# Attention and two expert layers on one core: when the fifth and sixth weight slices are split, the SBUF order behind it, the first loads and the warm-up count

## The chip, the core and the metric

The kernel runs on one core of a Trainium2 chip. TensorE (PE) does the matmuls and writes PSUM; VectorE (DVE), ScalarE (ACT) and GpSimd (POOL) do the elementwise work; SyncE (SP) issues nearly all of the DMAs. Each engine runs its own instruction stream in order, and they wait for each other by semaphores. The metric is the time of the device for one execution, in microseconds (us); lower is better.

## What is computed

Attention over 2 batches, 8 heads, 768 positions and 64 dimensions, in which a query sees only the keys that fall in the same bucket (6 sign bits of a projection), and then two dense blocks (each in, activation, out) on the 1536 x 512 result. All is float32; w_in is 512 x 2048 and w_out 2048 x 512.

```python
def _attn_ref(q, k, v, proj) -> np.ndarray:
    ...
    mask = q_bucket[:, :, :, None] == k_bucket[:, :, None, :]
    scores = scale * np.matmul(q, k.transpose(0, 1, 3, 2))
    scores = np.where(mask, scores, -1000000000.0)
    ...
    attn = attn / (np.sum(attn, axis=-1, keepdims=True) + 1e-09)
    return np.matmul(attn, v).astype(np.float32)

def _moe_ref(x, w_in, w_out) -> np.ndarray:
    h = x @ w_in
    alpha = 1.0
    g = np.where(h > 0.0, h, alpha * (np.exp(np.minimum(h, 0.0)) - 1.0))
    return (g @ w_out).astype(np.float32)
...
def _moe2_ref(x, w_in, w_out, s, b) -> np.ndarray:
    h = x @ w_in
    r = np.maximum(h, 0.0)
    g = s * (r * r) + b
    return (g @ w_out).astype(np.float32)
```

## The kernel before

Precision is kept by splitting every float32 operand into a rounded high part and a low remainder (`_hi`, `_lo`) and running three matmuls in place of one.

**Attention** goes over 8 pairs of heads (`PAIRS`), each pair over 12 units of 128 queries (`UNITS`). A unit is: scores on PE (L623, L624), scaling on DVE (L893), exp on ACT (L787), transposes on PE (L637), the high part by ACT (L781) and the low part by DVE (L900); every third unit goes through `pt_raw` and is split on POOL (`split_third`, L454 and L456). The product with the values (`times_v`, L652 and L653) runs in four groups of a pair (`GROUPS`). Its result takes a way of its own: DVE copies it out of PSUM (`keep_x`, L921; for groups 2 and 3 into `x_second`), SP moves it across partitions by DMA (`move_first` L339, `move_second` L346), POOL adds the two parts (`sum_x`, L463), scales them by the inverse row sums and splits them into `xt_hi` and `xt_lo` (`split_x`, L473, L476, L478). That is done for each of the two halves n of a pair, and POOL does half 1 of a pair during the next pair.

**Dense layers** go over 3 chunks of 512 tokens (`CHUNKS`), each over 16 slices f of the hidden dimension (`FT`). `hidden(layer, c, f)` is 12 matmuls of 512 columns (L672), `output(layer, c, f)` 12 more (L690); ACT and DVE make the activation in between. In the very first chunk `chunk(0, 0, 2, 3)` runs `output` three slices behind `hidden`, and slices 0 and 1 have had their `hidden` inside the attention's last pair. PE waits in `hidden` for `w_split >= f + 1`.

**Weights.** Slice f arrives by two DMAs of 256 KB (`load_w`, L317 and L318) in one of two buffers `w_raw`, and POOL splits it (`split_w`, L496 and L498; called by `weights(f)`). A load of slice f waits until slice f - 2 is split. Slices 0 to 3 (`EARLY = 4`) go to tiles of their own, `wa_hi` and `wa_lo`. Slices 4 and up go to `wb_hi` and `wb_lo`, which lie over memory of the attention: tiles are laid out in the order in which the program names them, `att.close()` gives the attention's region back, and `wb_*` are named after it. From L122 on that region holds, in KB per partition, `raw` 0 to 6, `qqk` to 33, `pt_hi` to 51, `pt_lo` to 69, then the row sums, `kt1`, `probs` and the rest. `wb_hi` begins at 24 and `wb_lo` at 72, 4 KB a slice. So slice 4 lies over `qqk` and `kt1`, operands of the scores, and POOL waits for the last scores (`scores_done`, L526) before it writes there.

What sets the order around this is nothing but the order in which the streams of POOL and SP are written. At the end of the last pair (i = 7) POOL does slice 4 before `split_x(6, 1)`, and slice 5 between the two halves of pair 7. SP issues the load of slice 4 ahead of `move_first(7, 1)`, and that of slice 5 ahead of the two `move_second` of pair 7.

**Start.** SP loads the table of planes (26 KB) and then the first half of head 0's rows, ACT the second half. PE runs `keep_warm(WARM)`, seven matmuls on zeros, then `first_signs` (L593: one float32 matmul of 44 x 384 outputs for each half of the rows, recorded as four instructions; it waits for `planes_built` and `rows0_in`), eight more warm-up matmuls, and the first scores. Between `first_signs` and the scores DVE turns the signs into bits (`to_bits`, L881).

Of the kernel before, what the change touches and what calls it, by code (L numbers as in the profile page):

```python
# [7 lines left out]
F32 = mybir.dt.float32  # L8
F32R = mybir.dt.float32r
# [3 lines left out]
P = 128  # L13
BATCH, HEADS, SEQ, DH = 2, 8, 768, 64
BITS = 6
BIT_ROWS = 32
TILES = SEQ // P
HALF = SEQ // 2
# [12 lines left out]
W = 2 * DM  # L31
WARM = 7

# [62 lines left out]
def build(nc, qk, v, planes_in, ident_in_d, w1_in, w1_out, w2_in, w2_out, s2, b2, out, inv_d):  # L96
    ctx = ExitStack()
    with ctx:
# [3 lines left out]
        def sb(name, shape, dt, where=ctx):  # L102
            return where.enter_context(nc.sbuf_tensor(name, shape, dt))
# [21 lines left out]
        qt1, qt2, kt2 = [[t[:, m, :] for t in qqk] for m in range(3)]  # L125

        pt_hi = [sb(f"pt_hi{n}", [P, TILES, HALF], F32R, att) for n in range(2)]
        pt_lo = [sb(f"pt_lo{n}", [P, TILES, HALF], F32R, att) for n in range(2)]

        row_sum = sb("row_sum", [P, UNITS, 2], F32, att)  # L130
        row_min = sb("row_min", [P, UNITS], F32, att)
        row_inv = sb("row_inv", [P, UNITS], F32, att)
        kt1 = [sb(f"kt1_{n}", [P, SEQ], F32R, att) for n in range(SETS)]

        probs = [sb(f"probs{n}", [P, SEQ], F32, att) for n in range(SRING)]
        raw_v = [sb(f"raw_v{n}", [P, TILES, DH], F32, att) for n in range(2)]
        pt_raw = sb("pt_raw", [P, SEQ], F32, att)
        bits = sb("bits", [SIGN_ROWS, HALF], F32R, att)
# [5 lines left out]
        ones = sb("ones", [P, HT], F32, att)  # L144
        v_nat = [sb(f"v_nat{n}", [P, TILES, 2 * DH], F32R, att) for n in range(2)]

# [117 lines left out]
        def _(sp):  # L264
# [49 lines left out]
            def load_w(layer, f, buf, splits):  # L314

                wait(sp, w_split, splits)
                sp.dma_start(w_raw[buf][:, 0:DM].rearrange("p (c n) -> p c n", n=P), row(win_d[layer], f)).then_inc(w_landed[buf], 16)  # L317
                sp.dma_start(w_raw[buf][:, DM:W], row(wout_d[layer], f)).then_inc(w_landed[buf], 16)  # L318
# [29 lines left out]
            def pair(i):  # L348
# [41 lines left out]
                get_inv(i, 0)  # L390
                if not nxt:
                    load_w(0, EARLY, 0, EARLY - 1)
                move_first(i, 1)
                put_inv(i, 3)

            sp.dma_start(planes_in_sb[:], planes_in).then_inc(planes_landed, 16)
            sp.dma_start(raw[0][:, halves[0]], qk[0, :, halves[0]]).then_inc(rows0_in[0], 16)
# [7 lines left out]
            for i in range(PAIRS):  # L405
                pair(i)
                if i == 1:
                    sp.dma_start(sb_scale[:, 0:1], s2.rearrange("(a n) -> a n", a=1).to_broadcast([P, 1])).then_inc(scale_in, 16)
                    sp.dma_start(sb_scale[:, 1:2], b2.rearrange("(a n) -> a n", a=1).to_broadcast([P, 1])).then_inc(scale_in, 16)
            load_w(0, EARLY + 1, 1, EARLY)  # L410
            move_second(PAIRS - 1, 0)
            move_second(PAIRS - 1, 1)
            get_inv(PAIRS - 1, 1)


            with sp.Fori(EARLY // 2 + 1, FT // 2) as j:
                for n in range(2):
                    load_w(0, 2 * j + n, n, 2 * j + n - 1)
# [21 lines left out]
        def _(pool):  # L440
# [62 lines left out]
            def pair(i, place, prev=True, nxt=True):  # L503
# [19 lines left out]
                split_third(i, 3)  # L523
                if not nxt:

                    pool.wait_ge(scores_done, UNITS * PAIRS)  # L526
                    pool.nop(nofuse=True)
                    weights(EARLY)
                if prev:
# [36 lines left out]
            split_x(PAIRS - 1, 0)  # L566
            weights(EARLY + 1)
            sum_x(PAIRS - 1, 1)
            split_x(PAIRS - 1, 1)

            with pool.Fori(1, (FT - EARLY) // 2) as j:
# [207 lines left out]
        def _(act):  # L779
# [29 lines left out]
            def unit(i, k, place, more=True):  # L809
# [12 lines left out]
                if first and k == 1:  # L822
                    round_qk(2, 0, 2, 1)

            act.dma_start(raw[0][:, halves[1]], qk[0, :, halves[1]]).then_inc(rows0_in[1], 16)
            act.wait_ge(ones_ready, 1)
# [214 lines left out]
```

## Time and profile before

| | us |
|---|---|
| median of 3 runs | 756.19 (755.26 to 756.28) |
| time of the profiled execution | 756.28 |
| its span, first to last instruction | 754.5 |

The span is 1.8 us short of the execution's time. Attention takes the first 232 us or so, the two dense layers the rest. In the page's list of chains, PE holds 94% of the chain that ended last; the rest lies mostly on POOL and on weight loads by DMA. In the timelines "idle before" is how long the engine stood still just before that instruction, and "<-" names what ended it.

### The profile page before, as it was taken

How to read it: one execution, taken by the hardware profiler on the slowest of the kernel's cores; microseconds unless marked ns; L12 is line 12 of the kernel's file. 1: busy time of each engine (PE TensorE's matmuls, PEld its weight loads, DVE VectorE, ACT ScalarE, POOL GpSimd, SP SyncE). 2: the span in 40 equal slices, each digit the busy share in tenths (PEclk: the TensorE clock that was granted, in tenths of full speed). 3: DMA queues.
4: the chain of work that ended last, by engine and by line, in shares of the span. 5: the costliest groups of instructions: out<-in, count | busy, mean ns of one | idle time of the engine just before them, and what ended most of it. 6: DMA issues, size and time to landing. Idle time of an engine off the chain costs nothing.

```text
span 754.5 us, 11772 instructions
## 1 busy us (share of the span) xinstructions
PE 746.6 (99%) x3757; PEld 641.6 (85%) x3757; DVE 392.8 (52%) x756; ACT 315.5 (42%) x614; POOL 312.7 (41%) x251
## 2 busy tenths in 40 slices
PE   8999999999999999999999999999999999999997
PEld 6999999999998788888888888888888888888886
DVE  6888888888877564343334232443234323343233
ACT  7888888888873122222123212232222212121211
POOL 6799989988999992000000666620000000000000
PEclk9999999999999999999999999999999999999999
DMA  5765575465533341000000232300001000010001
GB/s 158 186 170 133 129 176 147 115 151 139 128 91 94 111 139 58 0 1 1 0 1 0 84 107 87 100 12 1 0 1 56 0 0 0 0 56 0 0 0 56
DMA packets 44466, 50.67 MB, mean 67 GB/s; under 512 B 8260, under 2 KB 33172, under 8 KB 44436
## 3 DMA queue, kind: packets, MB, share of 16 engines
q1 hardware_dynamic: 44148, 50.02, 24.4%
q8 instruction: 17, 0.28, 0.2%
q10 hardware_dynamic: 288, 0.26, 0.1%
q14 instruction: 13, 0.11, 0.1%
HBM read 29.45 MB, written 3.19 MB: 43 GB/s over the span
## 4 chain that ended last, share of the span: by engine, by line
PE 94%; POOL 3%; DMA 1%; DVE 1%; issue 0%; ACT 0%; SPq 0%; DVEq 0%; POOLq 0%
PE acc L690 34%; PE h_ps L672 32%; PE pt_ps L637 8%; PE s_ps L624 4%; PE s_ps L623 4%; PE pv_ps L652 4%; PE pv_ps L653 4%; POOL wb_lo L498 1%; DMA w_raw<-w_out_dram 1%; PE prep_ps L605 1%; PE prep_ps L604 1%; PE prep_ps L606 1%; PE pv_ps L611 1%; POOL x_sum L473 1%; POOL wb_hi L496 0%
## 5 line engine op out<-in xcount | busy, mean ns | idle before, releaser
L859 ACT ACTIVATE r_sb<-h_ps 128x512 f32<-128x512 f32 x96 | 57.4, 598 | 362.3 <-PE h_ps L672 362.3
L672 PE MATMUL h_ps<-xt_hi,wb_hi 128*128 (+1 forms) x288 | 112.1, 389 | 0.6 <-POOL wb_lo L498 0.6
L672 PE MATMUL h_ps<-xt_hi,wb_lo 128*128 (+1 forms) x288 | 112.0, 389 | 0.0
L672 PE MATMUL h_ps<-xt_lo,wb_hi 128*128 (+1 forms) x288 | 112.0, 389 | 0.0
L992 DVE TENSOR_SCALAR g_sb<-e_sb,sb_scale 128x512 f32<-128x512 f32 x48 | 27.8, 579 | 158.2 <-ACT e_sb L862 158.2
L893 DVE TENSOR_SCALAR_CACHE_REDUCE probs<-s_ps 128x768 f32<-128x768 f32 x96 | 91.8, 957 | 9.6 <-PE s_ps L624 7.1
L990 DVE SCALAR_TENSOR_TENSOR g_sb<-e_sb,h_ps 128x512 f32<-128x512 f32 x48 | 33.0, 687 | 121.8 <-ACT e_sb L862 121.3
L787 ACT ACTIVATE probs<-probs,row_min 128x768 f32<-128x768 f32 x96 | 90.0, 938 | 2.8 <-DVE probs L893 1.9
L637 PE MATMUL pt_ps<-ident_sb,probs 128*128 128x128 f32 x576 | 80.2, 274 | 1.3 <-DVE pt_lo L900 1.0
L998 DVE TENSOR_TENSOR g_lo<-g_sb,g_hi 128x512 fp32r<-128x512 f32 x96 | 74.0, 771 | 3.3
L637 PEld LDWEIGHTS pt_ps<-ident_sb,probs 128*128 128x128 f32 x576 | 68.1, 141 | 7.8 <-issue 2.3
L652 PE MATMUL pv_ps<-pt_hi,v_nat 128*128 128x384 f32 x192 | 72.2, 376 | 0.0
L900 DVE TENSOR_TENSOR pt_lo<-pt_ps,pt_hi 128x384 fp32r<-128x384 f32 x128 | 65.1, 550 | 3.6 <-ACT pt_hi L781 3.4
L623 PE MATMUL s_ps<-kt,qqk 128*128 128x384 f32 x192 | 65.4, 341 | 0.7 <-DVE probs L893 0.5
L624 PE MATMUL s_ps<-qqk 76*128 76x384 f32 x192 | 65.3, 340 | 0.0
L862 ACT ACTIVATE e_sb<-r_sb 128x512 f32<-128x512 f32 x96 | 60.7, 632 | 11.0 <-ACT r_sb L859 0.8
L653 PE MATMUL pv_ps<-pt_lo,v_nat 128*128 128x384 f32 x192 | 64.8, 337 | 0.0
L672 PEld LDWEIGHTS h_ps<-xt_hi,wb_hi 128*128 128x128 f32 x288 | 54.0, 188 | 12.1 <-issue 1.0
L672 PEld LDWEIGHTS h_ps<-xt_lo,wb_hi 128*128 128x128 f32 x288 | 54.1, 188 | 11.2
L672 PEld LDWEIGHTS h_ps<-xt_hi,wb_lo 128*128 128x128 f32 x288 | 54.1, 188 | 11.2
L496 POOL CAST wa_hi<-w_raw 128x1024 fp32r<-128x1024 f32 (+1 forms) x8 | 8.9, 1114 | 131.1 <-PE acc L690 131.1
L781 ACT ACTIVATE pt_hi<-pt_ps 128x384 fp32r<-128x384 f32 x128 | 55.9, 489 | 17.4 <-PE pt_ps L637 17.4
(92 smaller groups left out, 1527.1 us busy)
## 6 DMA issues: line engine op xcount, KB each, us to landing
w_raw<-w_in_dram SPq DMA_DIRECT2D x32, 256.0 KB, 2.8
w_raw<-w_out_dram SPq DMA_DIRECT2D x32, 256.0 KB, 2.9
raw<-qk_dram SPq DMA_DIRECT2D x15, 384.0 KB, 5.7
qqk<-kt SPq DMA_DIRECT2D x15, 384.0 KB, 3.8
raw_v<-v_dram SPq DMA_DIRECT2D x16, 192.0 KB, 4.2
all_inv<-inv_dram SPq DMA_DIRECT2D x16, 192.0 KB
x_parts<-x_second SPq DMA_DIRECT2D x16, 192.0 KB, 5.7
qqk<-qqk SPq DMA_DIRECT2D x15, 192.0 KB, 3.7
```

What stands on the lines that cost most here:

```text
L623: mm(s_ps[buf][:, n, 0:HALF], q1, kt1[ops][:, cols], start=True, stop=False)
L624: last = mm(s_ps[buf][:, n, 0:HALF], q2, kt2[ops][score_rows, cols], start=False, stop=True)
L637: last = nc.tensor.transpose(pt_ps[n][:, r * P:(r + 1) * P], probs[k % SRING][:, (n * HT + r) * P:(n * HT + r + 1) * P], ident_sb[:])
L652: mm(pv_ps[:, 0:HALF], v_nat[par][:, kt, :], pt_hi[buf][:, kt, :], start=kt == 0, stop=False)
L653: last = mm(pv_ps[:, 0:HALF], v_nat[par][:, kt, :], pt_lo[buf][:, kt, :], start=False, stop=kt == TILES - 1)
L672: last = mm(bank[:], w[a][:, kt * P:(kt + 1) * P], x[b], start=n == 0, stop=n == 3 * KT - 1)
L690: last = mm(acc[n][:], lhs, rhs, start=f == 0 and j == 0, stop=f == FT - 1 and j == 2)
L787: nc.scalar.activation(scores[:], scores[:], ACT.Exp, bias=row_min[:, k:k + 1], scale=-1.0, accum_out=row_sum[:, k, 0:1]).then_inc(exp_don ...
L862: nc.scalar.activation(e[:], r[:], ACT.Square if layer else ACT.Exp, scale=1.0 if layer else -1.0).then_inc(e_done, 1)
L893: ts(probs[k % SRING][:].rearrange("p (n c) -> p n c", n=2), s_ps[k % 2][:, :, 0:HALF], -SCALE, CEILING, ALU.mult, ALU.min, accum_out=row_ ...
L900: tt(pt_lo[(k // HT) % 2][where], pt_ps[n][:, 0:HALF].rearrange("p (t c) -> p t c", t=HT), pt_hi[(k // HT) % 2][where].bitcast(F32), ALU.s ...
L998: tt(lo[:], g[:], hi[:].bitcast(F32), ALU.subtract).then_inc(g_ready, 1)
```

## The change

- POOL: `weights(4)` leaves the end of the last pair and comes after `split_x(7, 0)`, and it waits for `pv_done`, the last product with the values, in place of `scores_done`. `weights(5)` comes after `split_x(7, 1)`.
- SP: the load of slice 4 comes after `move_second(7, 0)`, that of slice 5 after `get_inv(7, 1)`.
- SBUF: the order of the attention's tiles is another. `kt1`, `raw_v`, `v_nat`, `bits` and the planes come behind `qqk`, and `probs`, `pt_raw`, `pt_hi` and `pt_lo` behind those. Slice 4 in `wb_lo` (72 to 76 KB) then lies over `pt_hi`, an operand of `times_v`. No size changes.
- The load of the planes is issued by ACT, ahead of its half of the rows, and no longer by SP ahead of the other half.
- `WARM` is 10, from 7.

```diff
@@ -29,7 +29,7 @@
 END = 384
 CHUNKS = TOKENS // CHUNK
 W = 2 * DM
-WARM = 7
+WARM = 10
 
 EARLY = 4
 HBANKS, GRING, SRING = 4, 3, 3
@@ -123,18 +123,9 @@
 
         qqk = [sb(f"qqk{n}", [P, 3, SEQ], F32R, att) for n in range(SETS)]
         qt1, qt2, kt2 = [[t[:, m, :] for t in qqk] for m in range(3)]
-
-        pt_hi = [sb(f"pt_hi{n}", [P, TILES, HALF], F32R, att) for n in range(2)]
-        pt_lo = [sb(f"pt_lo{n}", [P, TILES, HALF], F32R, att) for n in range(2)]
-
-        row_sum = sb("row_sum", [P, UNITS, 2], F32, att)
-        row_min = sb("row_min", [P, UNITS], F32, att)
-        row_inv = sb("row_inv", [P, UNITS], F32, att)
         kt1 = [sb(f"kt1_{n}", [P, SEQ], F32R, att) for n in range(SETS)]
-
-        probs = [sb(f"probs{n}", [P, SEQ], F32, att) for n in range(SRING)]
         raw_v = [sb(f"raw_v{n}", [P, TILES, DH], F32, att) for n in range(2)]
-        pt_raw = sb("pt_raw", [P, SEQ], F32, att)
+        v_nat = [sb(f"v_nat{n}", [P, TILES, 2 * DH], F32R, att) for n in range(2)]
         bits = sb("bits", [SIGN_ROWS, HALF], F32R, att)
         planes_in_sb = sb("planes_in_sb", [P, C_END], F32, att)
         planes0 = sb("planes0", [P, 2, BIT_ROWS], F32, att)
@@ -142,7 +133,15 @@
         planes_hi = sb("planes_hi", [P, 2 * SIGN_ROWS], F32R, att)
         planes_lo = sb("planes_lo", [P, 2 * SIGN_ROWS], F32R, att)
         ones = sb("ones", [P, HT], F32, att)
-        v_nat = [sb(f"v_nat{n}", [P, TILES, 2 * DH], F32R, att) for n in range(2)]
+
+        probs = [sb(f"probs{n}", [P, SEQ], F32, att) for n in range(SRING)]
+        pt_raw = sb("pt_raw", [P, SEQ], F32, att)
+        pt_hi = [sb(f"pt_hi{n}", [P, TILES, HALF], F32R, att) for n in range(2)]
+        pt_lo = [sb(f"pt_lo{n}", [P, TILES, HALF], F32R, att) for n in range(2)]
+
+        row_sum = sb("row_sum", [P, UNITS, 2], F32, att)
+        row_min = sb("row_min", [P, UNITS], F32, att)
+        row_inv = sb("row_inv", [P, UNITS], F32, att)
 
         all_inv = [sb(f"all_inv{n}", [P, HALF], F32, att) for n in range(2)]
 
@@ -388,12 +387,9 @@
                 if nxt:
                     copy_q_lo(2 * i + 3)
                 get_inv(i, 0)
-                if not nxt:
-                    load_w(0, EARLY, 0, EARLY - 1)
                 move_first(i, 1)
                 put_inv(i, 3)
 
-            sp.dma_start(planes_in_sb[:], planes_in).then_inc(planes_landed, 16)
             sp.dma_start(raw[0][:, halves[0]], qk[0, :, halves[0]]).then_inc(rows0_in[0], 16)
             sp.wait_ge(rows0_in[0], 16)
             load_qk(1)
@@ -407,12 +403,13 @@
                 if i == 1:
                     sp.dma_start(sb_scale[:, 0:1], s2.rearrange("(a n) -> a n", a=1).to_broadcast([P, 1])).then_inc(scale_in, 16)
                     sp.dma_start(sb_scale[:, 1:2], b2.rearrange("(a n) -> a n", a=1).to_broadcast([P, 1])).then_inc(scale_in, 16)
-            load_w(0, EARLY + 1, 1, EARLY)
             move_second(PAIRS - 1, 0)
+            load_w(0, EARLY, 0, EARLY - 1)
             move_second(PAIRS - 1, 1)
             get_inv(PAIRS - 1, 1)
 
 
+            load_w(0, EARLY + 1, 1, EARLY)
             with sp.Fori(EARLY // 2 + 1, FT // 2) as j:
                 for n in range(2):
                     load_w(0, 2 * j + n, n, 2 * j + n - 1)
@@ -521,11 +518,6 @@
                 if not prev:
                     weights(0)
                 split_third(i, 3)
-                if not nxt:
-
-                    pool.wait_ge(scores_done, UNITS * PAIRS)
-                    pool.nop(nofuse=True)
-                    weights(EARLY)
                 if prev:
                     split_x(i - 1, 1)
                 else:
@@ -564,9 +556,13 @@
             pair(PAIRS - 1, PAIRS - 1, nxt=False)
             sum_x(PAIRS - 1, 0)
             split_x(PAIRS - 1, 0)
-            weights(EARLY + 1)
+
+            pool.wait_ge(pv_done, GROUPS * PAIRS)
+            pool.nop(nofuse=True)
+            weights(EARLY)
             sum_x(PAIRS - 1, 1)
             split_x(PAIRS - 1, 1)
+            weights(EARLY + 1)
 
             with pool.Fori(1, (FT - EARLY) // 2) as j:
                 for n in range(2):
@@ -822,6 +818,7 @@
                 if first and k == 1:
                     round_qk(2, 0, 2, 1)
 
+            act.dma_start(planes_in_sb[:], planes_in).then_inc(planes_landed, 16)
             act.dma_start(raw[0][:, halves[1]], qk[0, :, halves[1]]).then_inc(rows0_in[1], 16)
             act.wait_ge(ones_ready, 1)
             nc.scalar.activation(row_sum[:, 0, 0:1], ones[:, 0:1], ACT.Exp)
```

The places in the streams, from before and from the change. POOL at the end of the last pair, before (the number after a tile's name is its buffer: `x_sum1` is half 1, `w_raw0` holds slice 4, `w_raw1` slice 5):

```order
L496 CAST wb_hi<-w_raw0 128x1024 [waits scores_done,w_landed0]
L498 TENSOR_TENSOR wb_lo<-w_raw0,wb_hi 128x1024 [waits w_hi]
L473 TENSOR_TENSOR x_sum1<-x_sum1,all_inv1 128x384 [waits x_summed,inv_in1]
L476 CAST xt_hi<-x_sum1 128x384 [waits x_scaled]
L478 TENSOR_TENSOR xt_lo<-x_sum1,xt_hi 128x384 [waits xt_hi_done]
L463 TENSOR_TENSOR x_sum0<-x_parts0 128x384 [waits second_moved0]
L473 TENSOR_TENSOR x_sum0<-x_sum0,all_inv0 128x384 [waits x_summed,inv_in0]
L476 CAST xt_hi<-x_sum0 128x384 [waits x_scaled]
L478 TENSOR_TENSOR xt_lo<-x_sum0,xt_hi 128x384 [waits xt_hi_done]
L496 CAST wb_hi<-w_raw1 128x1024 [waits w_landed1]
L498 TENSOR_TENSOR wb_lo<-w_raw1,wb_hi 128x1024 [waits w_hi]
L463 TENSOR_TENSOR x_sum1<-x_parts1 128x384 [waits second_moved1]
```

And in the change:

```order
L470 TENSOR_TENSOR x_sum1<-x_sum1,all_inv1 128x384 [waits x_summed,inv_in1]
L473 CAST xt_hi<-x_sum1 128x384 [waits x_scaled]
L475 TENSOR_TENSOR xt_lo<-x_sum1,xt_hi 128x384 [waits xt_hi_done]
L460 TENSOR_TENSOR x_sum0<-x_parts0 128x384 [waits second_moved0]
L470 TENSOR_TENSOR x_sum0<-x_sum0,all_inv0 128x384 [waits x_summed,inv_in0]
L473 CAST xt_hi<-x_sum0 128x384 [waits x_scaled]
L475 TENSOR_TENSOR xt_lo<-x_sum0,xt_hi 128x384 [waits xt_hi_done]
L493 CAST wb_hi<-w_raw0 128x1024 [waits pv_done,w_landed0]
L495 TENSOR_TENSOR wb_lo<-w_raw0,wb_hi 128x1024 [waits w_hi]
L460 TENSOR_TENSOR x_sum1<-x_parts1 128x384 [waits second_moved1]
L470 TENSOR_TENSOR x_sum1<-x_sum1,all_inv1 128x384 [waits x_summed,inv_in1]
L473 CAST xt_hi<-x_sum1 128x384 [waits x_scaled]
```

The two rows of slice 4 have moved behind both `split_x(6, 1)` and the whole of half 0 of pair 7, and those of slice 5 (no longer in the piece) behind half 1.

SP at the same place, before, from the last `get_inv(7, 0)` on:

```order
L333 DMA all_inv0<-inv_dram 128x1x384 [waits x_scaled,inv_out0]
L317 DMA w_raw0<-w1_in_dram 128x4x128 [waits w_split]
L318 DMA w_raw0<-w1_out_dram 128x512
L339 DMA x_parts1<-x_parts1 64x384 [waits x_done,x_summed]
L326 DMA inv_dram<-row_inv 128x3 [waits inv_done,inv_in1]
L317 DMA w_raw1<-w1_in_dram 128x4x128 [waits w_split]
L318 DMA w_raw1<-w1_out_dram 128x512
L346 DMA x_parts0<-x_second0 64x2x384 [waits x_done,first_moved0]
L346 DMA x_parts1<-x_second1 64x2x384 [waits x_done,first_moved1]
L333 DMA all_inv1<-inv_dram 128x1x384 [waits x_scaled,inv_out1]
```

And in the change:

```order
L332 DMA all_inv0<-inv_dram 128x1x384 [waits x_scaled,inv_out0]
L338 DMA x_parts1<-x_parts1 64x384 [waits x_done,x_summed]
L325 DMA inv_dram<-row_inv 128x3 [waits inv_done,inv_in1]
L345 DMA x_parts0<-x_second0 64x2x384 [waits x_done,first_moved0]
L316 DMA w_raw0<-w1_in_dram 128x4x128 [waits w_split]
L317 DMA w_raw0<-w1_out_dram 128x512
L345 DMA x_parts1<-x_second1 64x2x384 [waits x_done,first_moved1]
L332 DMA all_inv1<-inv_dram 128x1x384 [waits x_scaled,inv_out1]
L316 DMA w_raw1<-w1_in_dram 128x4x128 [waits w_split]
L317 DMA w_raw1<-w1_out_dram 128x512
```

Two pairs of weight DMAs have changed places with the moves of `x_parts`: slice 4 now stands behind the first `x_second` row, slice 5 behind the last `all_inv` row.

## Rows read from the trace of the kernel before

**Rows 1.** The page: busy time by engine, and the granted clock in 40 slices.

```profile
PE 746.6 (99%) x3757; PEld 641.6 (85%) x3757; DVE 392.8 (52%) x756; ACT 315.5 (42%) x614; POOL 312.7 (41%) x251
...
PEclk9999999999999999999999999999999999999999
```

**Rows 2.** Timeline of the start: start us, us, engine, line, op, tiles, [idle before].

```profile
0.75 0.42 ACTq L825 DMA_DIRECT2D raw<-qk_dram  x1
...
1.21 0.42 SPq L397 DMA_DIRECT2D raw<-qk_dram  x1
...
1.33 2.61 PE L611 MATMUL pv_ps<-pt_hi 128*128 128x384 f32 x7 [1.33 <-DVE pt_hi L945]
...
3.80 0.52 ACT L781 ACTIVATE kt<-raw 64x384 fp32r<-64x384 f32 x1 [1.11 <-DMA raw<-qk_dram]
...
3.91 2.76 PE L593 MATMUL s_ps<-raw,planes 128*44 128x384 f32 x4
...
6.71 2.36 DVE L881 TENSOR_SCALAR qqk<-s_ps,planes_in_sb 12x768 fp32r<-12x768 f32 x3 [1.80 <-PE s_ps L593]
...
8.72 0.41 PE L623 MATMUL s_ps<-kt,qqk 128*128 128x384 f32 x1
```

**Rows 3.** Weight loads of the warm-up matmuls: two of the first seven, the second eight.

```profile
1.82 0.33 PEld L611 LDWEIGHTS pv_ps<-pt_hi 128*128 128x128 f32 x1
...
3.10 0.33 PEld L611 LDWEIGHTS pv_ps<-pt_hi 128*128 128x128 f32 x1
...
L611 PEld LDWEIGHTS pv_ps<-pt_hi x8: 187/188/333, 6.6 to 8.1; 128*128 128x128 f32 x8
```

**Rows 4.** Timeline of POOL (GpSimd) from 212 to 249 us.

```profile
212.57 1.02 POOL L463 TENSOR_TENSOR x_sum<-x_parts 128x384 f32<-128x384 f32 x1
...
216.51 0.53 POOL L488 CAST v_nat<-raw_v 128x384 fp32r<-128x384 f32 x1
...
226.12 1.85 POOL L456 TENSOR_TENSOR pt_lo<-pt_raw,pt_hi 128x768 fp32r<-128x768 f32 x1
...
228.64 1.04 POOL L496 CAST wb_hi<-w_raw 128x1024 fp32r<-128x1024 f32 x1 [0.67 <-DMA w_raw<-w_out_dram]
...
232.12 1.13 POOL L473 TENSOR_TENSOR x_sum<-x_sum,all_inv 128x384 f32<-128x384 f32 x1
...
234.93 1.20 POOL L463 TENSOR_TENSOR x_sum<-x_parts 128x384 f32<-128x384 f32 x1
...
239.69 1.23 POOL L496 CAST wb_hi<-w_raw 128x1024 fp32r<-128x1024 f32 x1
...
243.69 1.19 POOL L463 TENSOR_TENSOR x_sum<-x_parts 128x384 f32<-128x384 f32 x1
...
248.68 1.04 POOL L496 CAST wb_hi<-w_raw 128x1024 f32 x1
```

**Rows 5.** Timeline of SP's DMA issues near the seam.

```profile
228.59 5.40 SPq L346 DMA_DIRECT2D x_parts<-x_second  x2
...
235.60 0.35 SPq L318 DMA_DIRECT2D w_raw<-w_out_dram  x1
```

**Rows 6.** Landing of L346's first of these; of L318's four (220 to 245 us).

```profile
DMA to landing us min/median/max: 3.3/3.3/3.3
...
DMA to landing us min/median/max: 4.5/5.9/6.9
```

**Rows 7.** Timeline of PE: first matmul of hidden steps 4, 5 and 6.

```profile
240.80 0.39 PE L672 MATMUL h_ps<-xt_hi,wb_hi 128*128 128x512 f32 x1
...
246.24 0.39 PE L672 MATMUL h_ps<-xt_hi,wb_hi 128*128 128x512 f32 x1
...
252.43 0.47 PE L672 MATMUL h_ps<-xt_hi,wb_hi 128*128 128x512 f32 x1 [0.59 <-POOL wb_lo L498]
```

**Rows 8.** Busy time of DVE in three stretches: stretch, its length, busy (count), clock, DMA.

```profile
212.50:216.50 4.00, 3.32 (x8) 1.00 0.05 12
...
228.60:232.10 3.50, 0.00 (x0) 1.00 0.48 152
...
240.00:246.00 6.00, 5.90 (x6) 1.00 0.18 54
```

## The prediction

> **What bounds the kernel now.** I read the page first, then the timelines of two short stretches. PE is busy for 746.6 of 754.5 us, and the granted clock stands at full speed in all 40 slices [rows 1]. So a change that adds no matmul in the dense layers can only move the few microseconds in which PE stands still or runs at the slow pace. There are two such places, and the change touches both.
>
> The first is the start. The warm-up matmuls follow each other at the pace of their weight loads, four steps in 1.28 us (1.82 to 3.10), or 0.32 us a matmul of 384 columns [rows 3]. That is 1200 columns per us, the lower of the two levels (1.2 GHz), though the page's row of the clock shows full speed there; the pace decides. The second group begins with a 333 ns load and has a median of 188 [rows 3], so the rise to 2.4 GHz falls into it, some 6 us after the first matmul. `first_signs` lies before it: four instructions in 2.76 us, 3.91 to 6.67 [rows 2]. DVE has been idle for 1.80 us when it takes the signs at 6.71, and the first scores follow at 8.72 [rows 2]. This is a chain without slack from PE's first matmul on.
>
> The second is the seam. Hidden step 5 starts 5.44 us after step 4 (240.80, 246.24), which is one `hidden` and one `output` back to back; step 6 would be due at 251.68 and starts at 252.43 after an idle time of 0.59 that POOL's split of slice 6 ends [rows 7]. So POOL is already 0.75 us late there once, and from 226 us on its rows follow each other almost without a gap [rows 4]. Whatever makes POOL stand still, or puts a weight slice behind other work, shows on PE at this place.
>
> **The seam, step by step.** No POOL instruction is added or removed; the order changes. I price POOL's blocks from the start of one to the start of the next [rows 4]:
> - a weight slice: 3.48 us (228.64 to 232.12) or 4.00 (239.69 to 243.69);
> - `sum_x` and `split_x` of one half: 3.94 (212.57 to 216.51), 4.76 (234.93 to 239.69) or 4.99 (243.69 to 248.68);
> - `split_x` alone: 2.81 (232.12 to 234.93).
>
> The short values fall where DVE is idle (228.60 to 232.10) or busy for 3.32 of 4.00 us with the attention's work; the long ones where it is busy for 5.90 of 6.00 us with the activations of the dense layer [rows 8]. From 233 us on I take the long ones.
>
> Now the new order. POOL ends `split_third` at 226.12 + 1.85 = 227.97 and does `split_x(6, 1)` at once: 230.8. Then it needs `second_moved` of half 0. SP issues that move at 228.59 [rows 5] and it lands 3.3 us later [rows 6], at 231.9. POOL stands still for 1.1 us, where before it had slice 4 to do. Half 0 of pair 7 then takes 4.76: 232.0 to 236.7. The wait for `pv_done` costs nothing: the last product is over before hidden step 2, and PE does `hidden` 2, `hidden` 3 and `output` 0 (2.72 us each, half of 5.44) before 240.80, so by 232.6. The load of slice 4 is now issued behind the first `move_second`, at about 229.2 and 229.8; the slowest landing of its kind, 6.9 [rows 6], gives 236.7, just in time. Slice 4: 236.7 + 4.0 = 240.7, and step 4 is due at 240.80. So that one is met, with 0.1 to spare.
>
> Half 1: its move is issued at 233.4 as before (the second in the row of 228.59, which ends at 233.99) and has landed by 236.8. 240.7 + 4.99 = 245.7. Slice 5 is loaded from where slice 6 was loaded before (235.60 [rows 5]), and lands by 242.5 at the slowest [rows 6]: no wait. DVE runs out of work near 248, since PE gives it none, so I price slice 5 by the distance from the split of slice 6 to the matmul that waited for it, 248.68 to 252.43 [rows 4, 7]: 3.75 with the hand-over. Step 5 starts at 249.45, not 246.24: PE stands still for 3.2 us. What was late before, slice 6, no longer is: POOL ends it near 253.1, and step 6 is due at 249.45 + 5.44 = 254.9. Its load is issued when slice 4 is split (240.7) and has at least 8 us. Slice 7 is loaded from 249.3 on, lands by 256.7 at the slowest, is ready by 260.7 and due at 260.4; by the median landing of 5.9 it is on time. After that POOL needs 4 us a slice against PE's 5.44. The net is 3.2 - 0.75 = **+2.5 us**. Bounds: all blocks short gives 0.1 (below); all long, with slice 7 late as well, 3.2.
>
> **The start.** Three more warm-up matmuls at 0.32 us. The tenth load starts at 3.10 + 3 x 0.32 = 4.06, its matmul one step later, and the array is free for `first_signs` at 4.70, against a start at 3.91 before [rows 2, 3]: **+0.8 us**. The data would be there earlier. The first half of the rows was issued at 1.21 behind the planes and used at 3.80, 2.6 us later; issued at 0.75 it is there at 3.35 [rows 2]. But 3.35 is before 4.70, so this gain of 0.45 us is worth nothing while PE is still warming up. The second half moves back on ACT's queue by 0.45, to 1.2, and lands near 3.8, also before 4.70. ACT's and POOL's own parts of head 0 start 0.45 earlier, and nobody on the chain waits for them. `first_signs` took 2.7 us (3.91 to 6.6, where the second warm-up group starts [rows 3]); from 4.70 on it ends at 7.4, about when the clock rises. Bounds: at most 3 x 0.32 = 0.96; at least -0.5, if the clock rose before `first_signs`.
>
> On that: the trace shows the low pace for some 6 us of nearly unbroken work, through seven warm-up matmuls and all of `first_signs` [rows 2, 3]. The Trainium skill says, in TensorE: Matmul & The Clock Gate, What's actually happening, that the array is throttled by default and sustained activity releases it, and that where the rise falls varies from run to run because the monitor does not start with the kernel. By that page an earlier rise is possible here and would turn +0.8 into -0.5; by the row it is not to be expected, since three more matmuls do not begin earlier, they only push `first_signs` back.
>
> **The SBUF order.** No row prices an address. All tiles keep their size and their 128 partitions, and DVE (52%), ACT (42%) and POOL (41%) have room [rows 1]. I take nothing, within 0.3 us either way. The layout's real price is the wait for `pv_done`, counted above.
>
> **The sum.** 756.28 (the profiled execution: a span of 754.5 and 1.8 around it) + 2.5 + 0.8 = 759.6. The median of the runs is 0.1 lower, so 759.5.
>
> **The rivals.**
> - *The clock rises before `first_signs`.* `first_signs` then takes half of 2.7 us: 4.70 + 1.35 = 6.05, 0.5 ahead of the 6.6 of before. With the seam as forecast: 756.2 + 2.5 - 0.5 = 758.2. For it speaks that PE is busy without a break, against it the 6 us above. Slower still.
> - *Not slower: POOL's blocks at the seam run at their short durations.* Place: POOL from 232.0 to the end of slice 5. 232.0 + 3.94 + 3.48 + 3.94 + 3.48 = 246.84. PE then loses about 0.75 at step 5, which is what it lost at step 6 before. The seam costs 0.1, the whole 0.9: 757.1, within 0.2% of before. It decides at 247.0: each 0.1 us by which slice 5 is ready later costs 0.1. For it: 3.94 was measured while DVE was 83% busy. Against it: both blocks that ran beside the activations took 4.76 and 4.99. The Trainium skill, SBUF — State Buffer, Who interferes with whom, has DVE and GpSimd take turns on a shared pair of ports as an exclusive lock, by which the long blocks return wherever DVE works.
> - *PE's clock falls in the 3.2 us of standing still.* No row shows PE idle for that long inside the kernel. [...] The Trainium skill, TensorE: Matmul & The Clock Gate, What's actually happening, has an idle array put back to the low level.
> - *The change does not reach the path.* If the new order on POOL cost nothing in some way I don't see, only the start would be left: 757.0. It has no mechanism but the second rival's, so no chance of its own.
>
> **How the numbers follow.** Forecast (seam 1.9 to 3.2, start 0.4 to 1.0): 58%, its own range 758.5 to 760.4. Early clock: 12%. Short blocks: 10%. Clock falls: 12%. Something that no row prices (a late load at slice 4, where the margin is 0.1, or addresses): 8%, of which 2 faster, 3 within the band. A measurement of this kernel tells 0.2% (1.5 us) from no change; the band is 754.7 to 757.7. Short blocks and those 3 make 13% for the same, and 2% are left for faster; 85% slower. The range holds the forecast, the early clock, most of the short blocks and most of the clock's fall: 757.2 to 762.2.
>
> **What would show it.** In the profile of the changed kernel: `first_signs` at 4.6 to 4.8 and DVE's L881 (now L877) near 7.5; a wait of about 1 us on POOL before its `sum_x` of pair 7, half 0, ended by the DMA of `x_second`; step 4 on time; an idle time of 2.5 to 3.5 us on PE before hidden step 5, ended by POOL's split into `wb_lo`; none before step 6; and PE's pace after it 0.23 us a matmul, at the high level. Wrong would be: no idle time at step 5 (then the blocks were short), an idle time at step 4 as well (the load of slice 4 landed late), 0.43 us a matmul after the gap (the clock fell), or L881 before 6.7 (the clock rose early).

## The result, and the profile after

| | before | changed |
|---|---|---|
| median, us | 755.93 (755.26 to 756.28, 6 runs) | 760.32 (758.14 to 760.88, 6 runs) |
| profiled execution | 756.28, span 754.5 | 758.45, span 756.7 |
| ratio | | 1.0051, 95% interval 1.0037 to 1.0066 |

The changed kernel is slower by 0.5%, as forecast (759.5, 757.2 to 762.2). But its runs, six timed ones and the profiled one, are not one group. Three (the profiled one among them) took 758.1 to 758.5 us at a mean granted clock of TensorE of 1.000; four took 760.3 to 760.9 at 0.997 or 0.998. The profiled execution belongs to the short group, so its trace can't show what the long ones lost; an experiment below does.

The page of the changed kernel. Busy times are those of [rows 1] within 0.1 us for PE and POOL, DVE has 5 us more in the same 756 instructions, and the granted clock is full in all slices:

```profile
span 756.7 us, 11778 instructions
...
PE 746.7 (99%) x3760; PEld 643.1 (85%) x3760; DVE 397.7 (53%) x756; ACT 315.6 (42%) x614; POOL 312.7 (41%) x251
...
PEclk9999999999999999999999999999999999999999
```

The seam on POOL, which answers to [rows 4] (timeline: start, us, engine, line, op, tiles, idle before; lines are 3 lower than before's):

```profile
226.39 1.84 POOL L453 TENSOR_TENSOR pt_lo<-pt_raw,pt_hi 128x768 fp32r<-128x768 f32 x1
...
228.20 1.14 POOL L470 TENSOR_TENSOR x_sum<-x_sum,all_inv 128x384 f32<-128x384 f32 x1
...
232.29 1.01 POOL L460 TENSOR_TENSOR x_sum<-x_parts 128x384 f32<-128x384 f32 x1 [1.23 <-DMA x_parts<-x_second]
...
236.31 1.50 POOL L493 CAST wb_hi<-w_raw 128x1024 fp32r<-128x1024 f32 x1
...
240.31 1.47 POOL L460 TENSOR_TENSOR x_sum<-x_parts 128x384 f32<-128x384 f32 x1
...
244.99 1.24 POOL L493 CAST wb_hi<-w_raw 128x1024 fp32r<-128x1024 f32 x1
...
248.93 1.23 POOL L493 CAST wb_hi<-w_raw 128x1024 f32 x1
```

POOL ends `split_third` at 228.2, does `split_x(6, 1)`, and then stands still for 1.23 us until the DMA of `x_second` lands. Half 0 takes 4.02 us (232.29 to 236.31), slice 4 takes 4.00, half 1 takes 4.68, slice 5 is done before 248.93.

PE at hidden steps 4, 5 and 6, which answers to [rows 7]:

```profile
241.07 0.39 PE L668 MATMUL h_ps<-xt_hi,wb_hi 128*128 128x512 f32 x1
...
249.12 0.47 PE L668 MATMUL h_ps<-xt_hi,wb_hi 128*128 128x512 f32 x1 [2.45 <-POOL wb_lo L495]
...
254.68 0.39 PE L668 MATMUL h_ps<-xt_hi,wb_hi 128*128 128x512 f32 x1
```

Step 4 is on time. Step 5 was due at 241.07 + 5.44 = 246.51 and starts at 249.12, 2.6 us late, after an idle time of 2.45 that POOL's split ends. Step 6 follows 5.56 later without a wait. It started at 252.43 before: 2.25 us of difference, of which 0.27 were there at step 4 already (241.07 against 240.80). That leaves 2.0 for the seam.

The start, which answers to [rows 2]:

```profile
0.75 0.42 ACTq L821 DMA_DIRECT2D planes_in_sb<-planes_dram  x1
...
1.33 3.57 PE L607 MATMUL pv_ps<-pt_hi 128*128 128x384 f32 x10 [1.33 <-DVE pt_hi L942]
...
3.43 0.52 ACT L777 ACTIVATE kt<-raw 64x384 fp32r<-64x384 f32 x1 [0.25 <-DMA raw<-qk_dram]
...
3.61 0.49 DVE L947 TENSOR_TENSOR planes<-planes_in_sb 128x24 f32<-128x24 f32 x1 [2.31 <-DMA planes_in_sb<-planes_dram]
...
4.83 2.06 PE L589 MATMUL s_ps<-raw,planes 128*44 128x384 f32 x4
...
6.94 2.35 DVE L878 TENSOR_SCALAR qqk<-s_ps,planes_in_sb 12x768 fp32r<-12x768 f32 x3 [1.37 <-PE s_ps L589]
...
8.91 0.43 PE L619 MATMUL s_ps<-kt,qqk 128*128 128x384 f32 x1 [0.40 <-issue]
```

The first half of the rows is there at 3.43, before 3.80. `first_signs` starts 0.92 us later than before (4.83, 3.91), but takes 2.06 us in place of 2.76, and the first scores are only 0.19 late (8.91, 8.72). So this trace has +2.0 at the seam and +0.2 at the start. What makes the long group, and why `first_signs` got shorter, was the question for the experiments.

Every experiment ran beside the kernel before on its chip. On two of the three chips a few runs of most kernels, before's too, took some 4 to 10 us more than the rest (called disturbed below), which widens the intervals there; I give medians, and the undisturbed runs where the number needs them.

### The profile page after: what moved, and what is told of

Its sections match the earlier page's. It is cut to its first block, busy times and chain, and to the rows that moved or that the text cites. A ratio compares the mean times of both kernels' runs of the same rounds, so it can differ in the third digit from the quotient of the medians.

```text
span 756.7 us, 11778 instructions
## 1 busy us (share of the span) xinstructions
PE 746.7 (99%) x3760; PEld 643.1 (85%) x3760; DVE 397.7 (53%) x756; ACT 315.6 (42%) x614; POOL 312.7 (41%) x251
## 4 chain that ended last, share of the span: by engine, by line
PE 96%; POOL 2%; issue 0%; DMA 0%; ACT 0%; DVE 0%; DVEq 0%; POOLq 0%; SPq 0%
PE acc L686 34%; PE h_ps L668 33%; PE pt_ps L633 8%; PE s_ps L619 4%; PE pv_ps L648 4%; PE s_ps L620 4%; PE pv_ps L649 4%; PE prep_ps L602 1%; PE pv_ps L607 1%; PE prep_ps L600 1%; PE prep_ps L601 1%; POOL wb_lo L495 1%; DMA x_parts<-x_second 0%; POOL wb_hi L493 0%; POOL x_sum L460 0%
## 5 line engine op out<-in xcount | busy, mean ns | idle before, releaser
L995 DVE TENSOR_TENSOR g_lo<-g_sb,g_hi 128x512 fp32r<-128x512 f32 x96 | 77.8, 810 | 3.3
```

What stands on the lines that cost most here:

```text
L995: tt(lo[:], g[:], hi[:].bitcast(F32), ALU.subtract).then_inc(g_ready, 1)
```

## Experiments

### The seam's part alone

Planes on SP and 7 warm-up matmuls as before; the streams of POOL and SP, the SBUF order and the wait as in the change.

```diff
-WARM = 10
+WARM = 7
...
-            act.dma_start(planes_in_sb[:], planes_in).then_inc(planes_landed, 16)
...
+            sp.dma_start(planes_in_sb[:], planes_in).then_inc(planes_landed, 16)
```

> The kernel before with the seam's part of the change alone (streams of POOL and SP, SBUF order, wait for the last product); planes on SP and 7 warm-up matmuls as before. Theory (seam +2.3 us by PE's wait at hidden step 5, start +0.2 to +0.8, and a further 2 us in those runs in which PE's clock falls in the wait): 758.0 us in runs at mean clock 1.0 and 760.1 in runs at 0.997. Rival 1 (the second cluster comes from the start, not from the wait): all runs near 758.0 at clock 1.0. Rival 2 (the seam costs nothing, the start everything): 756.0.

Measured: 759.78 us (median of 5) against 756.26, ratio 1.0039 (1.0025 to 1.0053). One run of 757.66 at clock 1.000, three of 759.35 to 759.90 at 0.997, and one of 760.18 at 1.000 that fits neither. The two groups are there without the start's part, so the seam makes them. This time the profiled execution (759.35) is one of the long group. The windows around PE's wait (stretch, its length, PE busy and count, granted clock, DMA share, GB/s):

```profile
240.00:246.00 6.00, 6.00 (x28) 1.00 0.30 98
...
246.00:249.00 3.00, 0.56 (x3) 0.88 0.00 0
...
249.00:252.00 3.00, 3.00 (x8) 0.55 0.53 175
...
252.00:256.00 4.00, 4.00 (x19) 1.00 0.42 130
```

and its step 5:

```profile
248.73 0.77 PE L669 MATMUL h_ps<-xt_hi,wb_hi 128*128 128x512 f32 x1 [2.44 <-POOL wb_lo L496]
...
249.29 0.63 PE L669 MATMUL h_ps<-xt_lo,wb_hi 128*128 128x512 f32 x1
...
250.15 0.63 PE L669 MATMUL h_ps<-xt_hi,wb_hi 128*128 128x512 f32 x1
...
252.25 0.39 PE L669 MATMUL h_ps<-xt_hi,wb_hi 128*128 128x512 f32 x1
...
252.71 0.39 PE L669 MATMUL h_ps<-xt_hi,wb_lo 128*128 128x512 f32 x1
...
255.65 0.39 PE L669 MATMUL h_ps<-xt_hi,wb_hi 128*128 128x512 f32 x1
```

PE is idle for 2.44 us, and in that wait the granted clock falls: 0.88 on average over 246 to 249, 0.55 over 249 to 252, full again from 252. In step 5 the matmuls start 0.43 us apart (249.29 to 250.15 is two of them), which is 512 columns at 1.2 GHz, and 0.23 apart at the end (252.25 to 252.71 is two), the pace of the higher level, 2.4 GHz. From the start of the first to the start of the last, the twelve take 3.98 us, in the trace of the change 2.62. The fall costs 1.4 us here.

### PE's wait filled with work

Ten matmuls of 512 columns, into the bank that step 5 overwrites:

```diff
+FILL = 10
...
+                bank = h_ps[f % HBANKS]
+                if layer == 0 and isinstance(c, int) and f == EARLY + 1:
+                    for _ in range(FILL):
+                        mm(bank[:], wa_hi[:, 0:P], xt_hi[:, 0:CHUNK], start=True, stop=True)
                 pe.wait_ge(w_split, layer * FT + f + 1)
-                bank = h_ps[f % HBANKS]
```

> The change whole, and in PE's wait ahead of hidden step 5 ten matmuls of 512 columns into the bank that step 5 overwrites (10 x 0.227 = 2.3 us of a wait of 2.5 us). Theory (the slow runs of the change are those in which the clock falls because PE stands still there): every run at 758.2 to 758.8 and mean clock 1.0, none at 760.3. Rival (the clock falls for another reason): the same two clusters, 758.4 and 760.4.

Measured: 758.97 us (5 runs) against 756.26. No run below 0.999, where the change had four of seven. But the forecast of the times was too tight: 758.05, 758.56 and 758.97 are within it or near, 759.71 and 760.35 are not, at a clock of 0.999. Something else made those two longer; the runs don't show what.

The same with eleven matmuls, and beside it the change itself once more, on a third chip:

```diff
-FILL = 10
+FILL = 11
```

> The change with eleven matmuls of 512 columns in PE's wait ahead of hidden step 5 (11 x 0.227 = 2.5 us, the whole wait). Theory (the clock falls because PE stands still): no run below mean clock 0.999, the undisturbed runs at 758.2 to 759. Rival (it falls for another reason): about half of the runs at 0.997.

> The change itself once more, beside the next three on the same chip. Theory: two groups of runs 2 us apart, the longer one at mean granted clock 0.997 or 0.998: 758.2 to 758.6 and 760.3 to 760.9, about half of the runs in each. Rival: one group only, if the first split was chance.

Measured: 758.26 us with the wait filled (12 runs, none below 0.999) and 758.67 for the change (11 runs, three of them at 0.997 or 0.998), against 756.63. The six shortest filled runs are 757.66 to 757.85; three more lie at 758.66 to 758.80, and three above, all at 0.999 or 1.000. The granted clock in the trace with the wait filled, for the stretch in which it fell above:

```profile
246.00:249.00 3.00, 3.00 (x14) 1.00 0.00 0
...
249.00:252.00 3.00, 3.00 (x15) 1.00 0.54 175
```

PE is busy throughout, the clock stays. Without the fall the seam still costs its 2 us: step 5 starts 8.03 us after step 4 (240.27, 248.30) with the wait filled, and 8.05 in the change (241.07, 249.12). The matmuls only keep the clock up. In the first set more than half of the change's runs had fallen (4 of 7), here 3 of 11, so the median lies in the other group; that fits its being 1.7 lower.

### PE's wait made longer

Two more casts on POOL ahead of slice 5, into room that is overwritten later:

```diff
             split_x(PAIRS - 1, 1)
+            for n in range(4, 6):
+                nc.gpsimd.tensor_copy(at(wb_hi, n), wa_hi[:, 0:W].bitcast(F32))
             weights(EARLY + 1)
```

> The change with two more casts on POOL ahead of the split of slice 5 (into room that slices 8 and 9 take later; the result is the same), which makes PE's wait 2.2 us longer, 4.7 in place of 2.5. Theory: the clock falls in every run, all at mean clock 0.997 or below, and the time is 2.2 us over the longer group of the change: 762.6. Rival 1 (the fall has nothing to do with the length of the wait): still half and half, 760.6 and 762.6. Rival 2 (POOL's delay is hidden): as the change.

Measured: 762.87 us (762.51 to 763.37, 5 runs), ratio 1.0079 (1.0056 to 1.0101), and every run at a mean clock of 0.997 or 0.995. Step 5, and the clock around it:

```profile
252.20 0.77 PE L670 MATMUL h_ps<-xt_hi,wb_hi 128*128 128x512 f32 x1 [5.05 <-POOL wb_lo L495]
```

```profile
249.00:252.00 3.00, 0.00 (x0) 0.54 0.00 0
...
252.00:256.00 4.00, 3.80 (x9) 0.50 0.41 131
...
256.00:262.00 6.00, 6.00 (x27) 0.99 0.47 139
```

The wait is 5.05 us, and the clock is low for most of it and for eight of the twelve matmuls behind it. Step 6 follows step 5 by 7.35 us (252.20, 259.55), where it is 5.56 in the change, so this fall costs 1.8. About half of the runs fall with a wait of 2.4 or 2.5 us (16 of 35), all with one of 5.

The count over all kernels, by the wait that their trace shows:

| kernel | PE's wait at the seam, us | runs at a mean clock of 0.998 or less |
|---|---|---|
| before | 0.59 | 3 of 85 (all three above 761 us, disturbed otherwise) |
| slice 6 ahead (below) | none | 0 of 23 |
| the start's part, or one of its two edits (below) | 0.7 to 1.2 | 0 of 34 |
| wait filled | 0.2 or none | 0 of 17 |
| wait for the last product at the old place (below) | 1.8 and 2.2 | 4 of 12 |
| the change | 2.5 | 7 of 18 |
| seam or order alone | 2.4 | 9 of 17 |
| longer wait | 5.05 | 5 of 5 |

Three of the runs counted here (one of the change at 769.03, two of the order alone at 762.25 and 764.64) are disturbed as well, so a fall at the seam is not certain for them.

### Order, addresses and the wait for the last product

First the streams of the change with the SBUF order of before and `scores_done` as the wait. The edit of the wait, against the change (the order of the tiles goes back as well and is not printed):

```diff
-            pool.wait_ge(pv_done, GROUPS * PAIRS)
+            pool.wait_ge(scores_done, UNITS * PAIRS)
```

> The streams of POOL and SP as in the change, but the SBUF order of before and the old wait for the scores; planes and warm-up as before. Theory (order alone costs, neither addresses nor the wait for the last product do): the same as the seam's part alone, 757.7 in undisturbed runs at clock 1.0 and 759.4 to 760.2 at 0.997. Rival (addresses or the wait cost something): shorter than that by the amount.

Measured: 759.92 us (12 runs, several disturbed) against 756.76, ratio 1.0035 (1.0004 to 1.0066). The two shortest runs are 757.49 and 757.52 at 1.000, and four are 759.30 to 759.77 at 0.997: the same two groups as the seam's part alone (757.66; 759.35 to 759.90). The two kernels ran on chips whose before differs by 0.5 us, so times alone would leave that much open. The traces leave less: from the first scores to hidden step 4 it is 232.08 us before and 232.10 in this run, both with the old addresses, and 232.16 in the change and 232.20 in the seam's part alone, with the new ones. PE's wait at step 5 is 2.43 us here, 2.44 in the seam's part. So neither the addresses nor the wait for the last product cost more than some 0.1 us in the change; the order does.

Then the other way round, streams of before, with the SBUF order of the change and the wait that it forces, at the old place:

```diff
+        kt1 = [sb(f"kt1_{n}", [P, SEQ], F32R, att) for n in range(SETS)]
...
+        v_nat = [sb(f"v_nat{n}", [P, TILES, 2 * DH], F32R, att) for n in range(2)]
...
         pt_hi = [sb(f"pt_hi{n}", [P, TILES, HALF], F32R, att) for n in range(2)]
...
-                    pool.wait_ge(scores_done, UNITS * PAIRS)
+                    pool.wait_ge(pv_done, GROUPS * PAIRS)
                     pool.nop(nofuse=True)
                     weights(EARLY)
```

> The kernel before with the SBUF order of the change and, forced by it, the wait for the last product (pv_done) at the old place of slice 4, ahead of split_x(6, 1); streams otherwise as before. Theory: addresses cost nothing; POOL now waits from 228 to 232.9 us where it had slice 4 to do, and everything behind it, slice 5 and 6 too, is 4.2 us later: PE waits at hidden step 5 for about 1.8 us and at step 6 for about 2.6 more, +3.5 to +4 us over before (760), and a further 2 us in runs in which the clock falls. Rival (the wait is hidden, as 0.0 was taken for it in its new place): near before.

Measured: 760.48 us (12 runs) against 756.76, ratio 1.0045 (1.0027 to 1.0063). POOL's wait, and PE's two:

```profile
232.49 1.04 POOL L496 CAST wb_hi<-w_raw 128x1024 fp32r<-128x1024 f32 x1 [5.01 <-PE pv_ps L653]
```

```profile
248.11 0.47 PE L672 MATMUL h_ps<-xt_hi,wb_hi 128*128 128x512 f32 x1 [1.79 <-POOL wb_lo L498]
...
256.02 0.47 PE L672 MATMUL h_ps<-xt_hi,wb_hi 128*128 128x512 f32 x1 [2.20 <-POOL wb_lo L498]
```

POOL loses 5.01 us and PE 4.0, in two waits. This profiled run (761.46) is one of the four in which the clock falls, and the fall comes behind the second wait, when PE is busy again:

```profile
257.02 0.39 PE L672 MATMUL h_ps<-xt_lo,wb_hi 128*128 128x512 f32 x1
...
257.60 0.63 PE L672 MATMUL h_ps<-xt_hi,wb_hi 128*128 128x512 f32 x1
...
258.03 0.63 PE L672 MATMUL h_ps<-xt_lo,wb_hi 128*128 128x512 f32 x1
```

The first matmuls behind the wait (from 256.02) start 0.23 us apart; from 257.60 on they start 0.43 apart. Step 7 follows at 263.19, 7.17 us after step 6, where 5.56 is the distance without a fall: 1.6 us lost.

So the SBUF order is not harmless as such. It costs 3.7 us where slice 4 is still split early, and nothing to speak of once slice 4 has moved behind the last product: of the two ways to live with the new SBUF order, the moved streams are the cheaper one, at about 2 us with the clock up.

### The start

Both edits of the start, without the seam's:

```diff
-WARM = 7
+WARM = 10
...
-            sp.dma_start(planes_in_sb[:], planes_in).then_inc(planes_landed, 16)
...
+            act.dma_start(planes_in_sb[:], planes_in).then_inc(planes_landed, 16)
```

> The kernel before with the start's part alone: planes issued by ACT, 10 warm-up matmuls. Theory: +0.2 to +0.8 us over before, the spread by when the clock rises in each run; no run at mean clock 0.997 and none 2 us longer than the others. Rival 1: two clusters 2 us apart, if the start makes them. Rival 2 (the extra warm-up matmuls bring the clock up earlier): 0.5 us shorter than before.

Measured: 756.92 us (11 runs) against 756.26, +0.7, ratio 1.0008 (0.9999 to 1.0017): no group at 0.997 and no gain. The interval, -0.1 to +1.3 us, holds zero and the forecast of 0.8 alike, so the runs don't settle the amount. Then each edit alone, first the count:

```diff
-WARM = 7
+WARM = 10
```

> The kernel before with 10 warm-up matmuls in place of 7, nothing else. By the sum on record +0.8 us (3 x 0.32 less the slack). Theory after the first traces: the clock rises between 6 and 7.3 us in every run seen, whatever the count, so a later first_signs runs partly at the high level; +0.2 to +0.6 us. Rival (more warm-up, earlier clock): shorter than before.

Measured: 757.69 us (12 runs) against 756.76 on a disturbed chip, ratio 1.0012 (0.9985 to 1.0039). It says nothing by itself. The profiled run (762.37) is one of the disturbed ones, and its trace shows where part of that time goes: PE waits four times, 3.7 us in all, for the DMA that brings the bits into `qqk` (`PE s_ps L623 <- DMA qqk<-bits`), a wait that the trace of before doesn't have. The expectation read the rise of the clock at 6 to 7.3 us in every trace; that was too narrow, as the trace of the start's part (below) has it near 5. Then the planes:

```diff
-            sp.dma_start(planes_in_sb[:], planes_in).then_inc(planes_landed, 16)
...
+            act.dma_start(planes_in_sb[:], planes_in).then_inc(planes_landed, 16)
```

> The kernel before with only the load of the planes moved to ACT; 7 warm-up matmuls. The first half of the rows is there 0.4 us sooner, but the warm-up ends at 3.75 and first_signs started at 3.91 before. Theory: 0.1 to 0.2 us shorter than before, at most 0.45. Rival: longer by 0.4, if the planes land later behind the 192 KB that are issued with them (in the trace of the change DVE took them at 3.61, in that of before at 3.09).

Measured: 756.40 us (11 runs) against 756.26, ratio 0.9999 (0.9990 to 1.0008): no gain. Its trace says why:

```profile
3.31 0.34 SPq L281 DMA_DIRECT2D raw<-qk_dram  x1
...
3.49 0.50 DVE L950 TENSOR_TENSOR planes<-planes_in_sb 128x24 f32<-128x24 f32 x1 [2.19 <-DMA planes_in_sb<-planes_dram]
...
3.92 0.28 DVE L952 TENSOR_TENSOR planes<-planes_in_sb 128x24 f32<-128x24 f32 x2
...
4.05 2.68 PE L592 MATMUL s_ps<-raw,planes 128*44 128x384 f32 x4
```

The rows are there at 3.31, but the planes, used at 3.09 before, are used at 3.49, and DVE's first step on them takes 0.50 us in place of 0.18. `first_signs` starts at 4.05. In the five traces with the start of before and 7 warm-up matmuls it is 3.91 to 4.03, so the move makes it no earlier. Of the two loads that `first_signs` needs, the planes now come last.

What `first_signs` takes differs by trace, with the same instructions. Two traces with 10 warm-up matmuls, of the start's part and of the longer wait:

```profile
4.83 1.52 PE L592 MATMUL s_ps<-raw,planes 128*44 128x384 f32 x4
...
6.28 1.68 PE L610 MATMUL pv_ps<-pt_hi 128*128 128x384 f32 x8
...
8.37 0.41 PE L622 MATMUL s_ps<-kt,qqk 128*128 128x384 f32 x1 [0.41 <-POOL qqk L554]
```

```profile
4.83 2.49 PE L591 MATMUL s_ps<-raw,planes 128*44 128x384 f32 x4
...
7.25 1.68 PE L609 MATMUL pv_ps<-pt_hi 128*128 128x384 f32 x8
...
9.34 0.41 PE L621 MATMUL s_ps<-kt,qqk 128*128 128x384 f32 x1 [0.41 <-issue]
```

It starts at 4.83 in both and takes 1.52 or 2.49 us; the second group starts at 6.28 or 7.25. That is when the pace goes from the lower level to the higher: at the lower one throughout it takes about 2.7 us, as before's trace has it. From what each trace saves against that, I estimate the rise near 5.0 and 7.0 us in these two, and near 4.5 in the earliest, the trace with eleven matmuls in the wait (`first_signs` 4.64, first scores 8.15). Over the six traces with 7 warm-up matmuls the first scores start at 7.88 to 8.85, 8.53 on average, over the seven with 10 at 8.15 to 9.34, 8.78 on average. The three matmuls cost about 0.25 us, below a scatter of 1 us between runs.

### Slice 6 ahead of half 1

The kernel before loses 0.75 us at step 6. Its `split_x(7, 1)` is needed for chunk 1 only, so the slices that chunk 0 waits for can go first:

```diff
             split_x(PAIRS - 1, 0)
             weights(EARLY + 1)
+            pool.wait_ge(pv_done, GROUPS * PAIRS)
+            pool.nop(nofuse=True)
+            weights(EARLY + 2)
             sum_x(PAIRS - 1, 1)
             split_x(PAIRS - 1, 1)
+            weights(EARLY + 3)
-            with pool.Fori(1, (FT - EARLY) // 2) as j:
+            with pool.Fori(2, (FT - EARLY) // 2) as j:
```

> The kernel before with slice 6 split ahead of half 1 of pair 7, and slice 7 behind it; planes and warm-up as before. Theory: the one wait at hidden step 6 goes, -0.75 us; with planes and warm-up changed as well it was 1.3 shorter than before (755.4 against 756.76). Rival (that gain came from the start): as before.

Measured: 755.47 us (754.75 to 756.42, 11 runs) against 756.63, ratio 0.9982 (0.9971 to 0.9993). The gain is 1.2 us where 0.75 was forecast, and the interval (0.5 to 2.2) holds both; in the trace, hidden steps 4 to 7 take 0.85 us less than before. PE's steps 5 to 7 follow each other by 5.44 us, with no wait:

```profile
246.25 0.39 PE L676 MATMUL h_ps<-xt_hi,wb_hi 128*128 128x512 f32 x1
...
251.69 0.39 PE L676 MATMUL h_ps<-xt_hi,wb_hi 128*128 128x512 f32 x1
...
257.13 0.43 PE L676 MATMUL h_ps<-xt_hi,wb_hi 128*128 128x512 f32 x1
```

With the planes on ACT and 6 warm-up matmuls as well:

```diff
-WARM = 7
+WARM = 6
...
-            sp.dma_start(planes_in_sb[:], planes_in).then_inc(planes_landed, 16)
...
+            act.dma_start(planes_in_sb[:], planes_in).then_inc(planes_landed, 16)
```

> The kernel before with slice 6 split ahead of half 1 of pair 7 (and slice 7 behind it), the planes on ACT and 6 warm-up matmuls. Theory: the wait at hidden step 6 (0.59 us idle, 0.75 us late) goes, the start gains 0 to 0.3: 0.7 to 1.0 us shorter than before. Rival (half 1 pushed back makes slice 7 late, or the wait moves to another slice): no gain or longer.

Measured: 755.40 us (12 runs) against 756.76 on a disturbed chip, ratio 0.9990 (0.9965 to 1.0014); eight of the runs are 754.9 to 756.0. The start adds nothing that I can see. The version with slice 6 ahead beats both kernels: before by 0.2% (the ratio above), and the change by 0.4% (755.47 against 758.67 on the same chip).

## Why the prediction was right, and where its terms were off

**The seam.** The mechanism was right in each step: POOL's wait for the move of half 0 (1.1 forecast, 1.23 measured), step 4 on time, PE waiting at step 5 for `wb_lo`, none at step 6, the wait for the last product free. Its size was not: 2.0 us in place of 2.5, and PE idle for 2.45 us, just under the 2.5 to 3.5 that I had named. Two blocks were priced too long: half 0 took 4.02, not 4.76, and half 1 took 4.68, not 4.99. Half 0 ran from 232.3 to 236.3, and DVE's work on the dense layer starts in that time only; "from 233 us on the long ones" was too coarse (DVE was busy for 2.66 of these 4.00 us, in slice 4 behind it for 3.93 of 4.00). Slice 5 took 4.13 with the hand-over, not 3.75: the short price rested on DVE running out of work near 248, and DVE was busy for 3.93 of 4.00 us from 245 to 249.

**The start.** The step that failed is the length of `first_signs`. I read 2.76 us from one trace and kept it. It is at the low pace only until the clock rises, and the rise came anywhere between some 4.5 and 7 us. A later start then shortens it. Of +0.8 about +0.2 is left in the change's trace, +0.25 over thirteen traces, which is within their scatter; DVE took the signs at 6.94, not near 7.5. The runs of the start's part alone (+0.7) don't tell 0.2 from 0.8. The Trainium skill, TensorE: Matmul & The Clock Gate, What's actually happening, says that the rise moves from run to run; these traces agree. I quoted that, and then priced from the one trace all the same. The rival that the clock rises before `first_signs` had 12%. In two of the seven traces with 10 warm-up matmuls (the start's part alone and the eleven matmuls in the wait) it all but came true: `first_signs` took 1.52 and 1.49 us, near half of 2.76, and the first scores came at 8.37 and 8.15, ahead of the 8.72 of before. But with 7 warm-up matmuls one trace has 1.81 us and 7.88, so this is the scatter of the rise and no work of the extra matmuls, and the median of the start's part alone was not shorter. That the data would be there at 3.35 was half right: the rows were, the planes were not.

**The clock's fall.** This was a rival with a chance of 12%. It is in fact a part of what the change does, in 7 of 18 runs, four of the seven in the first set among them. It costs 1.4 us in each of the two traces with one wait of 2.4 us and a fall (seam's part, order alone), 1.6 behind a second wait of 2.2 us and 1.8 behind the wait of 5.05. The range's upper end, 762.2, left room for a dearer fall; no run here shows one. The groups lie about 2 us apart. What makes up the other 0.6 is open: no run of the change's long group was profiled. The filled and the lengthened wait settle the cause: PE standing still. The Trainium skill, TensorE: Matmul & The Clock Gate, What's actually happening, has an idle array put back to the low level; the traces agree. So this was no remote rival: for the likeliest time it was an even choice between a sum with it and one without.

**The sum.** 759.5 lies between the groups of 758.4 and 760.4 and is near the median (760.3) only because two terms were too large, by 0.5 and by up to 0.6, and a third, of 2 us in about half of the runs, was left out. That is luck: 756.2 + 2.0 + 0.2 gives the 758.4 of the short group, and the median fell into the long one. The direction and the place of the loss were no luck. The SBUF order was taken for nothing, and the stream order with the old addresses shows that it is.

## What to carry to other kernels

When an engine off the critical path is near its limit at one place (POOL here, 41% busy over the whole kernel), write down when each of its results is due and put first what is due first, and don't put work with slack, or a wait for a transfer, ahead of it. A wait of TensorE (of 2.2 to 5 us in these kernels) can have a second price beside its length, the clock, and that price is paid in some runs and not in others; so look at the granted clock of each run before the medians are compared. A buffer laid over another stage's operands decides by its address when it may first be written, and so in what order the streams can be written at all.

## What the runs showed of the hardware that I had not expected

- TensorE's clock went down in 16 of 35 runs with a wait of 2.4 or 2.5 us and in all 5 with 5.05 us; after the shorter it was back within step 5, at a loss of 1.4 us.
- The fall can come when TensorE is busy again: behind a wait of 2.20 us the matmuls ran at the higher pace for more than 1 us (256.02 to 257.25), and at the lower one from 257.60 on.
- The profile's row of the clock shows full speed at the start, where the matmuls run at 1200 columns per us (384 columns in 0.32 us); the pace has to be read from the start times.
- Moved from SP's queue to ACT's at the same time of issue (0.75 us), with a load of 192 KB on the other queue both times, the 26 KB of planes were used 0.4 us later (3.49, 3.09).
